# Attention and two MoE layers in one kernel: spaced-out weight pieces, a different top-2 pick, one float16 product for token numbers

## The chip, the cores and the metric

The kernel runs on one core of a Trainium2 chip. The metric is the device time of one execution in microseconds (us). The core has TensorE (PE), VectorE (DVE), ScalarE (ACT), GpSimd (POOL) and SyncE (SP), and 16 DMA engines. SP, ACT and POOL have each a queue from which they issue DMAs.

## The reference, cut to what matters

```python
# attention: block 32, window 16; 16 heads of 768 x 64
scores_l = scale * q @ k.T            # only |i - j| < 16
scores_s = scale * q @ k_sum.T + log(32)   # 24 block maxima of k
a = softmax([scores_l, scores_s]); x = a @ [v, v_sum]  # v_sum: block means of v
# MoE: 1536 tokens, 8 experts, top 2
logits = x @ w_gate
noise_scale = np.log1p(np.exp(x @ w_noise))
noisy_logits = logits + noise_scale * noise
top2 = np.argpartition(-noisy_logits, 2, axis=1)[:, :2]
# out[token] = sum over its two experts of weight * (relu(x @ w1[e]) @ w2[e])
# then a dense layer: h = x @ w_in; out = max(0.01 * h, h) @ w_out
```

## The kernel before

**Attention** goes over 8 pairs of heads (n = 0 to 7), each in three groups, so 24 steps c = 3n + g. In a step TensorE computes scores (`score`), turns the softmax output of the step before (`turn_probs`, L1231) and multiplies with the values of an earlier one (`weigh`, L1252); VectorE does maximum and normalisation, ACT exp. The values of a pair lie in `v_win`, one of three buffers. SP loads their windows (`load_windows`, L343); TensorE then takes block means of them inside a score step (`block_means`, L1200), VectorE copies these out, ACT issues three small DMAs that put them into rows (`mean_rows`, L689), and GpSimd copies the rows into `v_win` (L575). `weigh` of a pair's first group waits for that copy. For pair 7 the window is loaded at SP's step n = 5, the means belong to c = 19, and `weigh(21)` waits for GpSimd's copy. At the end come the turns of x for the gate, the last `turn_probs(23)`, `weigh(22)`, `weigh(23)` and the logits.

**SP's queue** is written out by hand. Beside its loads for pair n it issues the weight pieces of `PIECES_BESIDE[n]`; (e, c) is piece c of expert e, 512 KB, for experts 0 and 1 only. At even n it stores pair n - 1 of x, three stores of 256 KB each; pair 7 is stored last. A DMA gives its piece to whoever splits it into a high and a low part: GpSimd for expert 0 (`split_first`) and for pieces 3 and 7 of expert 1, and for the other six ACT (high part, L740), TensorE (difference by identity products, `second_low_part`, L1374 and L1375) and ACT again (low part out of PSUM, L746).

**Routing** follows the last logits (L961). VectorE computes softplus from exp and log of ACT, adds it to the logits, takes the eight largest of each token and tile (L991), then their indices (L994), and makes the one-hot `chosen` from them (L996). Running counts per expert (L1001) go to TensorE, which sums them over partitions: the counts (L1382) and the ranks (L1385, L1387; their bank also holds the third low part, so they wait for ACT's copy of it). TensorE runs the low parts 0 to 2 ahead of the counts and 3 and 4 behind the ranks. VectorE derives each token's slot (L1009 to L1025), tile and row of it, and compares with tile and row numbers: `one_tile`, two digits of the token number in `at_tile`, and `at_row` in four parts (L1034). 48 products of TensorE with them (24 copies by two digits, L1394) give `token_of`, the list of tokens per slot. Each part of `at_row` is waited for. Then TensorE does the last low part and 14 transposes of an identity (`keep_warm`).

**Tiles.** GpSimd gathers x by `token_of` (L605, L601); the tile loop over 31 tiles turns x (L1408), ACT casts the high part (L786), VectorE subtracts for the low part (L1064), and TensorE multiplies high by high, low by high and high by low (L1421). Tile 0 also waits for all six low parts of expert 1. After the tiles comes the dense layer. The instructions after the tile loop's start are the same in number before and after the change.

On VectorE `link` makes the next instruction wait for the one just issued; an instruction without it is followed at once.

## Time and profile before

| what | value |
|---|---|
| median of 3 runs | 790.65 us (790.47 to 792.28) |
| the profiled execution | 787.81 us |
| its span | 786.2 us |
| PE busy | 758.4 us (96%) |
| DVE, ACT, POOL busy | 264.1, 230.0, 368.7 us |
| HBM read, written | 75.43 MB, 23.59 MB |

Times inside the span are counted from its start. The profiled execution is one of its own, 2.84 us below the median of the runs. A busy TensorE is not TensorE at its peak, as its matmuls are pipelined. A releaser in square brackets is what ended the idle time before an instruction.

### The profile page before, as it was taken

How to read it: one execution, taken by the hardware profiler on the slowest of the kernel's cores; microseconds unless marked ns; L12 is line 12 of the kernel's file. 1: busy time of each engine (PE TensorE's matmuls, PEld its weight loads, DVE VectorE, ACT ScalarE, POOL GpSimd, SP SyncE). 2: the span in 40 equal slices, each digit the busy share in tenths (PEclk: the TensorE clock that was granted, in tenths of full speed). 3: DMA queues.
4: the chain of work that ended last, by engine and by line, in shares of the span. 5: the costliest groups of instructions: out<-in, count | busy, mean ns of one | idle time of the engine just before them, and what ended most of it. 6: DMA issues, size and time to landing. Idle time of an engine off the chain costs nothing.

```text
span 786.2 us, 13127 instructions
## 1 busy us (share of the span) xinstructions
PE 758.4 (96%) x4505; PEld 620.9 (79%) x4506; DVE 264.1 (34%) x481; ACT 230.0 (29%) x384; POOL 368.7 (47%) x313
## 2 busy tenths in 40 slices
PE   7887798999999999999999999999999999999998
PEld 6666656778888888888888888888888888888886
DVE  2787563212222122121221212245433334332223
ACT  3777562222221222212212122144222222222212
POOL 5488525568788787868388871920010001000000
PEclk8999899999999999999999999999999999999999
DMA  9989734994443725353353621462010101010001
GB/s 177 211 196 244 238 135 126 347 317 148 141 166 99 234 94 207 100 173 120 133 184 112 225 80 43 118 203 79 28 55 27 54 1 53 0 53 0 0 1 53
DMA packets 77041, 97.74 MB, mean 124 GB/s; under 512 B 45768, under 2 KB 49008, under 8 KB 76976
## 3 DMA queue, kind: packets, MB, share of 16 engines
q1 hardware_dynamic: 58832, 45.52, 20.9%
q0 software_dynamic: 12464, 43.79, 17.4%
q10 hardware_dynamic: 5712, 7.99, 2.7%
q8 instruction: 21, 0.34, 0.2%
q14 instruction: 12, 0.10, 0.0%
HBM read 75.43 MB, written 23.59 MB: 126 GB/s over the span
## 4 chain that ended last, share of the span: by engine, by line
PE 89%; DVE 4%; DMA 3%; ACT 2%; issue 1%; POOL 0%; ACTq 0%; SPq 0%; DVEq 0%; POOLq 0%
PE p L1421 43%; PE p L1507 6%; PE p L1509 6%; PE p L1508 6%; PE p L1522 5%; PE p L1524 5%; PE p L1523 5%; PE p L1413 3%; DMA v_win<-in_v 2%; PE p L1408 2%; PE p L1231 1%; ACT scores L659 1%; PE p L1252 1%; DMA mean_rows<-mean_parts 1%; DVE scores L869 1%
## 5 line engine op out<-in xcount | busy, mean ns | idle before, releaser
L558 POOL TENSOR_TENSOR w_lo<-stage,w_hi 128x1024 fp32r<-128x1024 f32 x56 | 134.2, 2396 | 4.7
L1421 PE MATMUL p<-w_hi,xT_hi 128*128 x248 | 99.3, 400 | 1.9 <-DVE xT_lo L1064 1.9
L1421 PE MATMUL p<-w_lo,xT_hi 128*128 x248 | 96.7, 390 | 0.0
L1421 PE MATMUL p<-w_hi,xT_lo 128*128 x248 | 96.7, 390 | 0.0
L1421 PE MATMUL p<-w_hi,hT_hi 128*128 x240 | 96.5, 402 | 0.0
L1421 PE MATMUL p<-w_lo,hT_hi 128*128 x240 | 93.9, 391 | 0.0
L1421 PE MATMUL p<-w_hi,hT_lo 128*128 x240 | 93.5, 390 | 0.0
L645 POOL DMA_INDIRECT y_pick<-y_by_tile,slots x20 | 19.2, 959 | 157.5 <-PE p L1494 132.4
L1507 PE MATMUL p<-f_xT_hi,w_hi 128*128 (+2 forms) x200 | 77.2, 386 | 0.8 <-DVE f_xT_lo L1108 0.8
L1509 PE MATMUL p<-f_xT_hi,w_lo 128*128 (+2 forms) x200 | 76.2, 381 | 0.0
L1508 PE MATMUL p<-f_xT_lo,w_hi 128*128 (+2 forms) x200 | 76.2, 381 | 0.0
L789 ACT CAST hT_hi<-p 128x1024 fp32r<-128x1024 f32 x30 | 30.5, 1015 | 154.9 <-PE p L1413 154.9
L1522 PE MATMUL p<-w_hi,f_hT_hi 128*128 128x512 f32 x192 | 74.8, 390 | 0.1
L1523 PE MATMUL p<-w_lo,f_hT_hi 128*128 128x512 f32 x192 | 74.7, 389 | 0.0
L1524 PE MATMUL p<-w_hi,f_hT_lo 128*128 128x512 f32 x192 | 74.7, 389 | 0.0
L1116 DVE SCALAR_TENSOR_TENSOR f_h<-p,f_h 128x512 f32<-128x512 f32 x48 | 33.2, 691 | 119.9 <-ACT f_h L819 119.9
L1064 DVE TENSOR_TENSOR xT_lo<-p,xT_hi 128x512 fp32r<-128x512 f32 x31 | 21.4, 691 | 149.7 <-ACT xT_hi L786 149.7
L784 ACT ACTIVATE h_row<-p 128x1024 f32<-128x1024 f32 x30 | 30.8, 1027 | 136.3 <-PE p L1421 136.3
L819 ACT COPY f_h<-p 128x512 f32<-128x512 f32 x48 | 28.2, 588 | 143.2 <-PE p L1509 143.2
L556 POOL TENSOR_SCALAR w_hi<-stage 128x1024 fp32r<-128x1024 f32 x56 | 59.1, 1056 | 16.1 <-DMA stage<-in_moe_w 13.4
L1070 DVE COPY y_row<-p 128x512 f32<-128x512 f32 x31 | 21.5, 694 | 115.9 <-PE p L1421 115.9
L1421 PEld LDWEIGHTS p<-w_hi,xT_hi 128*128 128x128 f32 x248 | 46.6, 188 | 11.0 <-issue 2.4
(227 smaller groups left out, 1283.4 us busy)
## 6 DMA issues: line engine op xcount, KB each, us to landing
stage<-in_moe_w POOLq DMA_DIRECT2D x48, 512.0 KB, 4.0
w_land<-in_moe_w SPq DMA_DIRECT2D x16, 512.0 KB, 6.8
y_by_tile<-y_row ACTq DMA_DIRECT2D x29, 256.0 KB, 2.0
x_by_tile<-x_ring SPq DMA_DIRECT2D x28, 256.0 KB, 5.0
x_row<-x_by_tile SPq DMA_DIRECT2D x28, 256.0 KB, 2.9
v_win<-in_v SPq DMA_DIRECT2D x8, 384.0 KB, 5.4
x_tokens<-x_out SPq DMA_DIRECT2D x12, 256.0 KB, 7.1
out<-f_y SPq DMA_DIRECT2D x9, 256.0 KB, 2.0
```

The costliest lines, as they stand in the source:

```text
L556: pool.tensor_scalar(w_hi[:, par, cols], stage[:, c % STAGES, :], 1.0, 1.0, ALU.mult, ALU.mult).then_inc(hi_split, 1)
L558: pool.tensor_tensor(w_lo[:, par, cols], stage[:, c % STAGES, :], w_hi[:, par, cols].bitcast(F32), ALU.subtract).then_inc(lo_split, 1)
L784: nc.scalar.activation(h_row[:], h_bank[:], ACT.Relu).then_inc(h_ready, 1)
L789: nc.scalar.copy(hT_hi[:].rearrange("p c m -> p (c m)"), hT_bank[:]).then_inc(hT_hi_ready, 1)
L1116: nc.vector.scalar_tensor_tensor(out=h, in0=f_h_bank[c % 2], scalar=0.01, in1=h, op0=ALU.mult, op1=ALU.max).then_inc(f_leaky_done, 1)
L1421: last = nc.tensor.matmul(bank, a, w, start=(c == 0 and i == 0), stop=(c == left_hi.shape[1] - 1 and i == 2))
L1507: nc.tensor.matmul(to, hi, f_xT_hi[:, cols], start=(k == 0), stop=False)
L1508: nc.tensor.matmul(to, hi, f_xT_lo[:, cols], start=False, stop=False)
L1509: last = nc.tensor.matmul(to, lo, f_xT_hi[:, cols], start=False, stop=(k == KD - 1))
L1522: nc.tensor.matmul(f_y_bank[m], f_hT_hi[:, c % 2, rows], hi, start=(c == 0), stop=False)
L1523: nc.tensor.matmul(f_y_bank[m], f_hT_hi[:, c % 2, rows], lo, start=False, stop=False)
L1524: last = nc.tensor.matmul(f_y_bank[m], f_hT_lo[:, c % 2, rows], hi, start=False, stop=(c == FC - 1))
```

## The change

It has five parts.

- SP issues pieces (1,3) and (1,4) only when the window of pair 7 has landed, (1,0) to (1,2) between the three stores of pair 5, and (1,5) to (1,7) when pair 7's mean rows have landed, ahead of the stores of pair 7.
- Softplus: instead of dividing by (1 + t) - 1 with a guard against zero, it subtracts ((1 + t) - 1 - t) / (1 + t) from the log. One addition moves ahead of the wait for exp.
- The picks: instead of indices, an equality with the largest and second largest value over 192 columns, a correction for ties, a running count (scan) over the same, and a product that keeps the first match.
- Slots and token numbers: first slots by a shifted view of the sums (one subtraction less, one memset more); the token number is one float16 value, so `at_tile` is one tensor op and there are 24 products; `keep_warm` after them has 8 transposes.
- The first tile's product takes all terms with x's high part first, and waits for the low part only then.

```diff
-        PIECES_BESIDE = [((0, 0), (0, 1)), ..., ((0, 7), (1, 3), (1, 4)), ((1, 0), (1, 1), (1, 2)), ((1, 5), (1, 6), (1, 7))]
+        PIECES_BESIDE = [((0, 0), (0, 1)), ..., ((0, 7),), (), ()]
+        PIECES_BEHIND_V = (3, 4)
+        PIECES_BETWEEN_STORES = (0, 1, 2)
+        PIECES_BEHIND_MEANS = (5, 6, 7)
...
+                if n == PAIRS - 3:
+                    sp.wait_ge(v_loaded[(PAIRS - 1) % VBUF], last_v)
+                    for c in PIECES_BEHIND_V:
+                        load_piece(1, c)
                 if n >= 1 and n % 2 == 0:
                     for g in range(GROUPS):
                         store_x(n - 1, g)
+                        if n == PAIRS - 2:
+                            load_piece(1, PIECES_BETWEEN_STORES[g])
+            sp.wait_ge(means_loaded[(PAIRS - 1) % VBUF], 16 * MEAN_LOADS * ((PAIRS + 1) // VBUF))
+            for c in PIECES_BEHIND_MEANS:
+                load_piece(1, c)
...
+            link(nc.vector.tensor_tensor(te(7), plain, te(0), ALU.add))
             dve.wait_ge(exp_done, 1)
             nc.vector.tensor_scalar_add(row(3), row(2), 1.0).then_inc(exp1_done, 1)
             dve.wait_ge(exp1_done, 1)
-            link(nc.vector.tensor_scalar_add(row(5), row(3), -1.0))
-            link(nc.vector.tensor_scalar(row(6), row(5), 0.0, None, ALU.is_equal))
-            link(nc.vector.tensor_tensor(row(5), row(5), row(6), ALU.add))
-            link(nc.vector.reciprocal(row(5), row(5)))
-            link(nc.vector.tensor_tensor(row(5), row(5), row(2), ALU.mult))
-            link(nc.vector.tensor_tensor(te(5), te(5), noise_sb[:], ALU.mult))
-            link(nc.vector.tensor_tensor(te(7), plain, te(0), ALU.add))
+            nc.vector.scalar_tensor_tensor(out=row(5), in0=row(3), scalar=-1.0, in1=row(2), op0=ALU.add, op1=ALU.subtract)
+            link(nc.vector.reciprocal(row(6), row(3)))
+            link(nc.vector.tensor_tensor(row(5), row(5), row(6), ALU.mult))
             dve.wait_ge(ln_done, 1)
-            link(nc.vector.tensor_tensor(row(6), row(6), row(4), ALU.add))
-            link(nc.vector.tensor_tensor(row(6), row(6), row(5), ALU.mult))
+            link(nc.vector.tensor_tensor(row(6), row(4), row(5), ALU.subtract))
+            link(nc.vector.tensor_tensor(te(6), te(6), noise_sb[:], ALU.mult))
             link(nc.vector.tensor_tensor(row(7), row(7), row(6), ALU.add))
...
-            for t in range(NT):
-                last = nc.vector.max_index(top8_at[:, t, :], top8[:, t, :], te(7)[:, t, :])
-            link(last)
-            link(nc.vector.tensor_tensor(chosen[:], iota_e..., top8_at..., ALU.is_equal))
+            nc.vector.tensor_tensor(tok(1), top8[:, :, 0], top8[:, :, 1], ALU.is_equal)
+            link(nc.vector.tensor_tensor(is_top[:], te(7)..., tops..., ALU.is_equal))
+            link(nc.vector.tensor_tensor(is_top[:, 1, :, 0], is_top[:, 1, :, 0], tok(1), ALU.subtract))
+            link(nc.vector.tensor_tensor_scan(flat_of(tops_so_far), same_pick..., flat_of(is_top), 0.0, ALU.mult, ALU.add))
+            link(nc.vector.scalar_tensor_tensor(out=flat_of(chosen), in0=flat_of(tops_so_far), scalar=1.0, in1=flat_of(is_top), op0=ALU.is_equal, op1=ALU.mult))
...
+            nc.vector.memset(tab_p[:, 2, 0:1], 0.0)
...
-            link(nc.vector.tensor_tensor_scan(g(2), ones[:, 0:E], g(1), 0.0, ALU.mult, ALU.add))
-            link(nc.vector.tensor_tensor(g(4), g(2), g(1), ALU.subtract))
+            link(nc.vector.tensor_tensor_scan(end_of, ones[:, 0:E], g(1), 0.0, ALU.mult, ALU.add))
...
-            nc.vector.tensor_tensor(at_tile[:, 0], one_tile[:], over(first_ids[:], TCOLS), ALU.mult)
-            nc.vector.tensor_scalar(at_tile[:, 1], one_tile[:], token_id[:, 0:1], None, ALU.mult)
+            nc.vector.tensor_tensor(at_tile[:], one_tile[:], over(token_ids[:], TCOLS), ALU.mult)
...
-                for digit in range(2):
-                    last = nc.tensor.matmul(token_bank, at_row[:, :, i], at_tile[:, digit, :, i], ...)
+                last = nc.tensor.matmul(token_bank, at_row[:, :, i], at_tile[:, :, i], start=(i == 0), stop=(i == 2 * NT - 1))
             last.then_inc(slots_done, 1)
             second_low_part(5)
-            keep_warm(14, p01[:, BANK:BANK + P])
+            keep_warm(8, p01[:, BANK:BANK + P])
...
+            def first_tile_product(w):
+                for half in range(2):
+                    for c in range(KD):
+                        hi, lo = w(c * F + 512 * half)
+                        for i, part in enumerate((hi, lo)):
+                            nc.tensor.matmul(h_bank[...], xT_hi[:, c, :], part, start=(c == 0 and i == 0), stop=False)
+                pe.wait_ge(xT_lo_ready, 1)
+                for half in range(2):
+                    for c in range(KD):
+                        last = nc.tensor.matmul(h_bank[...], xT_lo[:, c, :], w(c * F + 512 * half)[0], start=False, stop=(c == KD - 1))
+                return last
...
                 pe.wait_ge(w1_ready, loads)
-                pe.wait_ge(xT_lo_ready, t + 1)
-                first_product(w).then_inc(h_done, 1)
+                if age == 0:
+                    pe.wait_ge(xT_hi_ready, 1)
+                    first_tile_product(w).then_inc(h_done, 1)
+                else:
+                    pe.wait_ge(xT_lo_ready, t + 1)
+                    first_product(w).then_inc(h_done, 1)
```

The 16-bit tiles change from bfloat16 to float16. On GpSimd three small iotas at the start become one (`token_ids`), and the scan's mask `same_pick` is set by two memsets.

## Rows read from the trace of the kernel before

**Rows 1.** The page: busy us of TensorE (share of the span), instructions.

```profile
PE 758.4 (96%) x4505; PEld 620.9 (79%) x4506; DVE 264.1 (34%) x481; ACT 230.0 (29%) x384; POOL 368.7 (47%) x313
```

**Rows 2.** Timeline of SP's DMA issues, 50 to 130 us: start, us, what.

```profile
69.83 0.61 SPq L343 DMA_DIRECT2D v_win<-in_v  x1
...
85.56 1.61 SPq L350 DMA_DIRECT2D w_land<-in_moe_w  x3
```

**Rows 3.** Timeline, 64 to 106 us: start, us, engine, line, [idle before <-releaser].

```profile
79.34 1.20 PE L1200 MATMUL p<-v_win,half_sums 64*32 64x192 f32 x16 [2.87 <-DMA v_win<-in_v]
...
87.69 0.57 ACTq L689 DMA_DIRECT2D mean_rows<-mean_parts  x1
...
93.16 0.65 PE L1231 MATMUL p<-ident,scores 128*120 128x128 f32 x4 [0.22 <-ACT scores L659]
...
94.30 1.47 POOL L575 TENSOR_SCALAR v_win<-mean_rows 24x1536 f32<-24x1536 f32 x1 [7.34 <-DMA mean_rows<-mean_parts]
...
94.60 1.25 ACT L659 ACTIVATE scores<-scores,negmax 128x120 f32<-128x120 f32 x4 [0.17 <-DVE negmax L873]
...
95.83 0.69 PE L1252 MATMUL p<-v_win,probsT 120*64 120x65 f32 x16 [2.02 <-POOL v_win L575]
...
98.31 1.06 PE L1231 MATMUL p<-ident,scores 128*120 128x128 f32 x4
```

**Rows 4.** DMA queues of SP (q1) and ACT (q10): first 76:90, then 88:90.

```profile
q1 hardware_dynamic: 2314, 4.54, 97.8%
...
q10 hardware_dynamic: 1, 0.00, 0.1%
```

**Rows 5.** Windows: PE, PEld, DVE, ACT, POOL busy (count), then granted clock, DMA, GB/s.

```profile
98.00:99.00 1.00, 1.00 (x7) 0.97 (x5) 0.14 (x1) 0.44 (x1) 1.00 (x1) 0.50 0.00 0
...
125.00:126.00 1.00, 1.00 (x4) 0.48 (x2) 0.90 (x6) 0.00 (x0) 0.79 (x1) 0.50 0.00 0
```

**Rows 6.** Timeline of the routing, 106 to 128 us.

```profile
107.38 0.21 DVE L978 TENSOR_SCALAR r_sc<-r_sc 128x96 f32<-128x96 f32 x1
...
108.17 0.75 DVE L981 RECIPROCAL r_sc<-r_sc 128x96 f32<-128x96 f32 x1
...
110.71 0.92 DVE L991 MAX8 top<-r_sc 128x8 f32<-128x8 f32 x12
...
113.21 1.01 ACT L746 CAST w_lo<-p 128x1024 fp32r<-128x1024 f32 x1 [1.16 <-PE p L1375]
...
113.42 0.36 DVE L996 TENSOR_TENSOR chosen<-iota_e,top_at 128x192 f32<-128x192 f32 x1
...
114.17 0.36 DVE L1001 TENSOR_TENSOR_SCAN r_sc<-same_expert,r_sc 128x96 f32<-128x96 f32 x1
...
116.04 0.26 DVE L1016 TENSOR_TENSOR r_sc<-p,tab_p 128x96 f32<-128x96 f32 x1
...
119.05 0.41 DVE L1031 TENSOR_SCALAR at_tile<-one_tile,token_id 128x768 bf16<-128x768 bf16 x1
...
119.09 0.80 PE L1375 MATMUL p<-w_hi,minus_ident 128*128 128x512 f32 x1
119.37 2.17 DVE L1034 TENSOR_TENSOR at_row<-row_numbers,slot_b 128x768 bf16<-128x768 bf16 x4
...
119.98 3.53 PE L1394 MATMUL p<-at_tile,at_row 128*128 128x32 bf16 x48
...
124.62 1.16 POOL L605 DMA_INDIRECT x_first<-x_tokens,token_of  x1 [21.52 <-DVE token_of L1044]
...
127.28 1.01 ACT L746 CAST w_lo<-p 128x1024 fp32r<-128x1024 f32 x1 [4.81 <-PE p L1375]
```

**Rows 7.** The chain that ended last, around the first product.

```profile
128.96 0.45 PE p L1408 x4
...
130.05 0.70 DVE xT_lo L1064
...
131.00 5.76 PE p L1421 x24
```

More of the change, by code:

```diff
@@ L22 @@
 F32, F32R = mybir.dt.float32, mybir.dt.float32r
-I32, U32, BF16 = mybir.dt.int32, mybir.dt.uint32, mybir.dt.bfloat16
+I32, U32, F16 = mybir.dt.int32, mybir.dt.uint32, mybir.dt.float16
 ALU, ACT, AX = mybir.AluOpType, mybir.ActivationFunctionType, mybir.AxisListType
@@ L122, in build @@
         with ExitStack() as room:
[L123 to L125 removed]
+            row_numbers = sb("row_numbers", [P, P, 2 * NT], F16, where=room)
+            tile_numbers = sb("tile_numbers", [P, TCOLS, 2 * NT], F16, where=room)
+            token_ids = sb("token_ids", [P, 2 * NT], F16, where=room)
             before = sb("before", [P, P], where=room)
@@ L129, in build @@
             same_expert = sb("same_expert", [P, E, NT], where=room)
+            same_pick = sb("same_pick", [P, 2 * NT, E], where=room)
         stage = sb("stage", [P, STAGES, CW])
@@ L148, in build @@
         with ExitStack() as room:
-            sb("under_routing", [P, 2380], where=room)
+            sb("under_routing", [P, 2092], where=room)
             r_sc = sb("r_sc", [P, 12, NT * E], where=room)
@@ L501, in _ @@
             link(pool.memset(same_expert[:, :, 0], 0.0))
-            link(pool.iota(first_ids[:].rearrange("p (k t) -> p k t", k=2), [[0, 2], [P, NT]], base=0, channel_multiplier=0, allow_small_or_imprecise_dtypes=True))
+            link(pool.memset(same_pick[:], 1.0))
+            link(pool.memset(same_pick[:, :, 0], 0.0))
+            link(pool.iota(token_ids[:].rearrange("p (k t) -> p k t", k=2), [[0, 2], [P, NT]], base=0, channel_multiplier=1, allow_small_or_imprecise_dtypes=True))
             signal(pool.iota(tile_numbers[:], [[1, TCOLS], [0, 2 * NT]], base=0, channel_multiplier=0, allow_small_or_imprecise_dtypes=True))
@@ L992, in _ @@
             link(last)
-            for t in range(NT):
-                last = nc.vector.max_index(top8_at[:, t, :], top8[:, t, :], te(7)[:, t, :])
-            link(last)
-            link(nc.vector.tensor_tensor(chosen[:], iota_e[:].unsqueeze(1).unsqueeze(1).to_broadcast([P, 2, NT, E]),
-                                         top8_at[:, :, 0:2].rearrange("p t k -> p k t").unsqueeze(3).to_broadcast([P, 2, NT, E]), ALU.is_equal))
+            tops = top8[:, :, 0:2].rearrange("p t k -> p k t")
+            flat_of = lambda a: a[:].rearrange("p k t e -> p (k t e)")
+            nc.vector.tensor_tensor(tok(1), top8[:, :, 0], top8[:, :, 1], ALU.is_equal)
+            link(nc.vector.tensor_tensor(is_top[:], te(7).unsqueeze(1).to_broadcast([P, 2, NT, E]), tops.unsqueeze(3).to_broadcast([P, 2, NT, E]), ALU.is_equal))
+            link(nc.vector.tensor_tensor(is_top[:, 1, :, 0], is_top[:, 1, :, 0], tok(1), ALU.subtract))
+            link(nc.vector.tensor_tensor_scan(flat_of(tops_so_far), same_pick[:].rearrange("p a e -> p (a e)"), flat_of(is_top), 0.0, ALU.mult, ALU.add))
+            link(nc.vector.scalar_tensor_tensor(out=flat_of(chosen), in0=flat_of(tops_so_far), scalar=1.0, in1=flat_of(is_top), op0=ALU.is_equal, op1=ALU.mult))
             by_expert = lambda i: r_sc[:, i, :].rearrange("p (e t) -> p e t", e=E)
@@ L1034, in _ @@
                 nc.vector.tensor_tensor(at_row[:, :, copies], row_numbers[:, :, copies], over(slot_b[:, 1, copies], P), ALU.is_equal).then_inc(rows_known, 1)
-            link(nc.vector.tensor_scalar(g(5), g(2), 1.0 / P, None, ALU.mult))
+            link(nc.vector.tensor_scalar(g(5), end_of, 1.0 / P, None, ALU.mult))
             ft = lambda i: tab_f[:, i, 0:TILES]
@@ L1392, in _ @@
                     pe.wait_ge(rows_known, i // PART + 1)
-                for digit in range(2):
-                    last = nc.tensor.matmul(token_bank, at_row[:, :, i], at_tile[:, digit, :, i], start=(i == 0 and digit == 0), stop=(i == 2 * NT - 1 and digit == 1))
+                last = nc.tensor.matmul(token_bank, at_row[:, :, i], at_tile[:, :, i], start=(i == 0), stop=(i == 2 * NT - 1))
             last.then_inc(slots_done, 1)
             second_low_part(5)
-            keep_warm(14, p01[:, BANK:BANK + P])
+            keep_warm(8, p01[:, BANK:BANK + P])
             def turn_x(t, half=0, uses=0):
@@ L1427, in first_product @@
                     last = part_products(h_bank[:, 512 * half:512 * half + 512], range(KD), xT_hi, xT_lo, lambda c: w(c * F + 512 * half))
+                return last
[4 more added lines that the diff above has]
+                        for i, part in enumerate((hi, lo)):
+                            nc.tensor.matmul(h_bank[:, 512 * half:512 * half + 512], xT_hi[:, c, :], part, start=(c == 0 and i == 0), stop=False)
+                pe.wait_ge(xT_lo_ready, 1)
+                for half in range(2):
+                    for c in range(KD):
+                        last = nc.tensor.matmul(h_bank[:, 512 * half:512 * half + 512], xT_lo[:, c, :], w(c * F + 512 * half)[0], start=False, stop=(c == KD - 1))
                 return last
```

31 lines of the change are left out of this document (15 added, 16 removed).

## The prediction

> **What bounds the kernel now.** I began with the page: TensorE is busy for 96% of the span [rows 1]. A change pays only where TensorE waits, so I looked for its waits, and the list of waits and the chain of waits put nearly all of them ahead of the tile loop. From 131.00 us, where the first expert product starts [rows 7], TensorE hardly stops again, so what starts that product earlier moves the end by as much.
>
> Then the timeline of the end of attention. TensorE waits 2.87 us, until 79.34, for the last values' window, and 2.02 us, until 95.83, for GpSimd's copy of the last block means (L575), which itself waits for a DMA until 94.30 [rows 3]. That DMA was issued from ACT at 87.69, and in 88 to 90 one packet of its queue moved [rows 3, 4]. SP's queue was full: 4.54 MB in 76 to 90, 324 GB/s [rows 4]. The windows show the third cost: TensorE's granted clock is at 0.50, the 1.2 GHz level, in 98 to 99, after the second wait [rows 5].
>
> Last, the timeline of the routing, 106 to 131. It is a serial chain on VectorE, with TensorE beside it busy with the second expert's low parts; the two lists must be laid over each other, as the later one decides at each crossing.
>
> **Part 1, the paced pieces.** Ahead of the window load issued at 69.83 nothing changes in SP's order, and it is taken to be served in order: 9.5 us from issue to TensorE's start [rows 2, 3]. The first wait stays: 0. Behind it, three pieces (1,5) to (1,7), issued at 85.56 before [rows 2], come only after the means have landed. What is left behind the window: (0,7), mostly moved by 80.6, and then five pieces of 0.52 MB and three stores of 0.26 MB, 3.4 MB. By the 324 GB/s of [rows 4] that is 10.5 us from about 80.5: the queue is empty near 91 where it was empty near 94. The means then land near 91, GpSimd's copy of 1.47 us [rows 3] ends near 92.5, and TensorE reaches that product at 95.83 - 2.02 = 93.81. So the wait of 2.02 goes, with 1.3 us to spare. What is late next is the last softmax: TensorE's turn of it (L1231) waits for exps that ran from 94.60 for 1.25 [rows 3], so it starts at 95.9 and not 98.31: 2.4 us. Behind it the same work ran at the low clock (L1231 1.06 us, against 0.65 for the turn before [rows 3]); if the clock stays up, the transposes, this turn and the product after it give another 0.75. I take 3.15, because the low clock followed the wait; bounds 2.0 and 3.15.
> The moved pieces are covered: (1,5) is first read by ACT at 114, GpSimd reads (1,7) far later, and both would be in by 97. Pair 7's stores stand behind them on SP, but their data is ready only from 95.8. SP's new wait for the window holds up (1,3), (1,4) and the stores of pair 5, which nobody wants before 99. All 0.
>
> The Trainium skill, "DMA: Bandwidth & Descriptors", section "Queues, rings and completion order", says that an engine goes round-robin between its queue rows a packet at a time, so the SP backlog should hold the means up by a packet per turn and not by its whole length. The trace shows 6.6 us from the issue at 87.69 to the copy at 94.30 [rows 3]. By the rule alone part 1 would give less, which is the first rival.
>
> **Part 2, routing up to the counts.** Softplus: L978 to L980 took 107.38 to 108.17; now the moved add delays the start by 0.10 and one unlinked step of 0.18 follows, so the reciprocal (0.75) starts at 107.66, 0.51 earlier than 108.17 [rows 6]. From its start to L991's, 2.54 us, lay 0.79 for itself and six steps of 0.29; four are left: 0.58. L991 starts at 109.61, 1.10 earlier. Picks: from the end of L991 (111.63) to L996 (113.42) twelve index searches, 1.79, and L996, 0.36 with 0.04 of link, go. In come an is_equal over 12 values (0.10 unlinked), the is_equal over 192 (0.40, as L996), a fix on 12 (0.21), the scan over 192 and a product over 192 (0.40). The scan is not in the trace; over 96 it took 0.36 (L1001), a tensor op 0.26 (L1016), so per 96 values 0.10 more: 0.56 and a link 0.04 for 192. Bounds: 0.36 (no slower than L996) and 0.76. In all 1.71 for 2.19. The running counts, ready at 114.53, would be there 1.58 earlier, at 112.95.
> Here TensorE takes over. It is on the third low part until 113.17 (ACT's copy of it starts at 113.21 and lasts to 114.22 [rows 6]), so the count product starts at 113.2. The rank product wants that copy gone, as it writes the same bank: 114.3, and its two halves take 0.7, to 115.0. VectorE's table steps are over by 114.45, so the subtraction L1013 that goes and the memset that comes are hidden; if that cover were gone they would give 0.1 to 0.2. L1016 starts at 115.0 for 116.04: 1.04 gained, 0.75 of the 1.8 lost to TensorE and ACT.
>
> **Part 3, token numbers.** L1031 goes: 119.37 - 119.05 = 0.32. VectorE's row masks (L1034, 2.17 for four) then run 118.0 to 120.2. float16 is as wide as bfloat16, so I keep the durations; below that no reason for a gain, above it at worst L1034 twice as long, 2.2. TensorE's fourth and fifth low parts ended at 119.89 [rows 6]; they start with the ranks, 0.55 earlier, and end at 119.35. So the token product starts at 119.45, not at 118.6 when its first rows are known. It has 24 products and not 48: half of 3.53, 1.77. It ends at 121.2, when the last rows have been there for 1 us, and not at 123.51: 2.3 gained. GpSimd's first gather moves from 124.62 to 122.3; it was in before the turn of 128.96 [rows 7], so now by 126.6 at the latest.
> Then the sixth low part and the warming transposes, 8 for 14. Before, that part ended at 127.25 (ACT's copy starts at 127.28 [rows 6]), 3.74 us after the token product, at clock 0.50 in 125 to 126 [rows 5]. With the same 3.74 it ends at 124.95, ACT's copy at 126.0; fourteen transposes took 1.7, to 128.96 [rows 7], so eight take 1.0, to 125.95. The first tile's turn follows both, between 126.0 and 126.5. I take the later, as it waits for the copy's signal too: 2.5. Bounds: 2.9 if the clock stays up or the signal costs nothing, and 1.3 if it stays down through the transposes as well, each then twice as long.
>
> **Part 4, x's high part first.** The first product waited until 131.00 for xT_lo, which took 0.70 from 130.05, and 0.24 of signal [rows 7]. It now waits for xT_hi, which is there when xT_lo's work begins, and the same 0.24; the low products come after sixteen others, 3.8 us at 5.76 for 24, so xT_lo's 0.70 is covered by them: 0.7. The number of products is the same, and only for this tile.
>
> **Sum.** 3.15 + 2.5 + 0.7 = 6.35 us. The profiled execution took 787.81 us outside a span of 786.2; it becomes 781.5 (span 779.9). The runs' median is 790.65, 2.84 above; I take that distance as unchanged: 784.3. Nothing later gives it back as far as I see: the gathers for tile 3 on start with the token numbers too, 2.3 + 3.15 earlier.
>
> **The rivals.**
> 1. The means stay late, since the copy waits for the transfer's own turns among large packets and not for the backlog's end. For: the trace does not say which packets the means stood behind, and 3.4 MB are ahead of them still. Against: one packet in 88 to 90 [rows 4], and the landing at 94.30 just when the rest was through. Gain 3.2: 787.5.
> 2. The window load is not served in order, so the pieces behind it delayed it. Then the first wait of 2.87 and its low clock, some 1.5, go too: 779.9. Against: two pieces and three stores, 1.8 MB, stood ahead of it on SP (5.6 us at 324 GB/s), which with its own transfer fill the 9.5.
> 3. Routing gives little: the clock falls at another place, or ACT's copies decide. 0.9 for 3.2, total 4.0: 786.6.
> 4. Slower: with fewer warming transposes and a wait for the gather, the clock falls to 1.2 GHz as the first products begin. A tile's 24 products last 5.76 us [rows 7], 0.24 each; at half clock as much again. It turns the result when 27 products run low; over two tiles it is +11.5 - 6.35, or 795.8. Against: between the turn and the first product lay some 1.6 us without work before as well, and the products ran at 0.24, the high clock's pace.
> The Trainium skill, "TensorE: Matmul & The Clock Gate", says in its part on transposes that these do not count as busy for the clock gate in the same way. By it, 8 or 14 would matter little; the trace has the clock coming back during the 14, and no run here tells whether through them.
> 5. The change does nothing measurable, two parts falling short together: 789.5.
>
> **The numbers.** Forecast 0.62, rival 1 0.14, rival 2 0.06, rival 3 0.11, rival 4 0.03, rival 5 0.04. The forecast's own range by its bounds is 783.9 (3.15 + 2.9 + 0.7) to 786.7 (2.0 + 1.3 + 0.7). The range reaches past the lower for a partly shorter first wait and to rival 1: 782.4 to 787.6; it leaves out rivals 2, 4 and 5. No change is told from noise within 0.3%, 2.4 us: the forecast and rivals 1 to 3 are beyond it, rival 1 by 0.8 only, so part of it counts as same. Faster 0.89, same 0.08, slower 0.03.
>
> **What would show it.** In the changed profile: L1200's wait near 79.3 as before; no wait ahead of the third last L1252, with L575 starting near 91; a high clock in 94 to 98; L991 to the counts shorter by 0.5; the count product right behind a low part; 24 token products starting behind another low part; first product 6.3 us earlier, at 124.7. The prediction is wrong if the means still land at 94, or if a low clock stands over the first tiles.

## The result, and the profile after

The changed kernel takes 787.33 us, the median of 6 runs (785.75 to 787.85), against 790.64 us for the kernel before (790.32 to 792.28, 6 runs): the ratio over the runs is 0.9935, with a 95% interval of 0.9912 to 0.9959, or 3.2 to 7.0 us of 790.64. The medians alone are 3.3 us apart. The forecast was 784.3 with a range of 782.4 to 787.6, so the time lies at the range's upper end. The profiled execution took 787.29 us outside a span of 785.7; that of before took 787.81 and 786.2. These two profiles differ by 0.5 us, where the sum, made on the first, said 6.35. Where the rest went is the question of this part. The profile itself models the ends of TensorE's rows and does not measure them, which matters below.

The changed kernel's page, first part: busy us (share of the span), instructions. TensorE works 3.5 us less than in [rows 1].

```profile
PE 754.9 (96%) x4475; PEld 618.3 (79%) x4476; DVE 262.0 (33%) x457; ACT 230.0 (29%) x384; POOL 368.6 (47%) x313
```

The timeline of the changed kernel, SP's window load and the end of attention (start, us, engine, line; the lines are some 15 further down than before):

```profile
71.89 0.61 SPq L347 DMA_DIRECT2D v_win<-in_v  x1
...
80.98 0.86 PE L1215 MATMUL p<-v_win,half_sums 64*32 64x192 f32 x16 [2.09 <-DMA v_win<-in_v]
...
88.51 0.57 ACTq L704 DMA_DIRECT2D mean_rows<-mean_parts  x1
...
93.84 1.47 POOL L590 TENSOR_SCALAR v_win<-mean_rows 24x1536 f32<-24x1536 f32 x1 [4.59 <-DMA mean_rows<-mean_parts]
...
95.37 0.69 PE L1267 MATMUL p<-v_win,probsT 120*64 120x65 f32 x16 [0.73 <-POOL v_win L590]
...
97.16 0.60 PE L1246 MATMUL p<-ident,scores 128*120 128x128 f32 x4
...
104.07 0.26 DVE L976 TENSOR_TENSOR logits<-logits,p 128x96 f32<-128x96 f32 x1 [2.53 <-PE p L1312]
```

Against [rows 2, 3] the window load is issued 2.06 us later, before anything that the change touches. From there on things are sooner: TensorE's second wait is 0.73 us and not 2.02, and the turn L1246 takes 0.60 us and not 1.06. The last add to the logits starts 32.18 us after the window load's issue. In the kernel before that was 36.24 us (its row is below), so this stretch gave 4.06.

The windows of the same kernel (TensorE's busy us and count, granted clock, DMA share, GB/s). Nothing is at the low clock from 78 to 98 us, around the end of attention, but the first and the last row are:

```profile
12.00:20.00 8.00, 8.00 (x49) 0.50 1.17 193
...
78.00:98.00 20.00, 15.34 (x290) 1.00 0.74 248
...
132.00:134.00 2.00, 0.00 (x0) 1.00 0.90 306
134.00:142.00 8.00, 5.03 (x17) 0.57 0.99 328
```

The kernel before, the same kind of window near the start:

```profile
18.00:20.00 2.00, 2.00 (x30) 0.93 0.64 145
```

and, in its timeline, its last add to the logits and ScalarE's first write of h:

```profile
106.07 0.26 DVE L961 TENSOR_TENSOR logits<-logits,p 128x96 f32<-128x96 f32 x1 [2.53 <-PE p L1297]
...
136.78 1.02 ACT L784 ACTIVATE h_row<-p 128x1024 f32<-128x1024 f32 x1 [6.75 <-PE p L1421]
```

The row of 18 to 20 goes with the later start: before, TensorE was back at 2.4 GHz by then, in the changed kernel's execution it stood at 1.2 GHz until past 20. Apart from GpSimd's small tables at the start, the instructions up to there are the same in both. In the fourteen profiles of this study the window load's issue lies between 69.68 and 72.67 us with no order by kernel, and a second profile of the changed kernel has it at 70.05 us. These 2 us are chance.

The routing of the changed kernel, which answers to [rows 6]:

```profile
109.25 0.56 DVE L1010 TENSOR_TENSOR_SCAN tops_so_far<-same_pick,is_top 128x192 f32<-128x192 f32 x1
...
116.08 2.14 DVE L1049 TENSOR_TENSOR at_row<-row_numbers,slot_b 128x768 f16<-128x768 f16 x4
...
117.19 1.87 PE L1408 MATMUL p<-at_tile,at_row 128*128 128x32 f16 x24
...
120.17 1.16 POOL L620 DMA_INDIRECT x_first<-x_tokens,token_of  x1 [17.53 <-DVE token_of L1059]
```

The scan over 192 values, whose price the prediction had to guess, took the 0.56 us that it took for it. The 24 token products take 1.87 us. From the last logits to GpSimd's first gather it is 16.10 us, and was 18.55.

The chain that ended last, in the changed kernel, from the gather on:

```profile
120.17 3.49 DMA x_first<-x_tokens,token_of
...
125.30 3.93 PE p L1450 x16
129.23 1.82 PE p L1454 x8
...
131.49 5.48 issue
136.97 1.97 PE p L1427 x8
138.94 6.78 PE p L1435 x24
```

Here is the loss. In the kernel before the first product starts 24.93 us behind the last logits [rows 7], here 21.23, so 3.70 us more are won; all in all the first product starts at 125.30 and not at 131.00. But then 5.48 us pass with TensorE, by its rows, doing nothing, the eight transposes of h take 1.97 us, and the second tile's product starts at 138.94 and takes 6.78 us. Before, the transposes took 1.1 us, the second product started at 139.26 and took 5.75. Of 5.70 us ahead, 0.32 are left at its start.

The sum by stages, in us (both columns are profiled executions):

| stretch | before | after | gain | forecast |
|---|---|---|---|---|
| start to window load | 69.83 | 71.89 | -2.06 | 0 |
| window load to last logits | 36.24 | 32.18 | 4.06 | 3.15 |
| last logits to first product | 24.93 | 21.23 | 3.70 | 3.2 |
| first to second tile's product | 8.26 | 13.64 | -5.38 | 0 |

Behind it the second product costs 1.03 us more, and 1.36 come back at the entrance of the tile loop, where TensorE stood still in the kernel before (157.24 to 158.60) and does not here; that makes the 0.5 us of the spans within 0.2.

ScalarE waits for the same thing (the changed kernel's timeline, the rows of its engine):

```profile
124.46 0.59 ACT L801 CAST xT_hi<-p 128x512 fp32r<-128x512 f32 x1 [2.10 <-PE p L1422]
135.89 1.02 ACT L799 ACTIVATE h_row<-p 128x1024 f32<-128x1024 f32 x1 [10.85 <-remote]
```

The product's rows end at 131.05, and ScalarE, which waits for nothing but that end, starts at 135.89. "remote" says that the trace names nobody who ended the wait just then. Either the rows show a false end or ScalarE was held up by something else; the experiments had to say which.

### The profile page after: what moved, and what is told of

Its sections match the earlier page's. It is cut to its first block, busy times and chain, and to the rows that moved or that the text cites. A ratio compares the mean times of both kernels' runs of the same rounds, so it can differ in the third digit from the quotient of the medians.

```text
span 785.7 us, 13043 instructions
## 1 busy us (share of the span) xinstructions
PE 754.9 (96%) x4475; PEld 618.3 (79%) x4476; DVE 262.0 (33%) x457; ACT 230.0 (29%) x384; POOL 368.6 (47%) x313
## 4 chain that ended last, share of the span: by engine, by line
PE 90%; DMA 3%; DVE 2%; issue 2%; ACT 2%; POOL 0%; ACTq 0%; SPq 0%; POOLq 0%; DVEq 0%
PE p L1435 43%; PE p L1538 6%; PE p L1540 6%; PE p L1539 6%; PE p L1553 5%; PE p L1555 5%; PE p L1554 5%; PE p L1427 4%; DMA v_win<-in_v 2%; PE p L1422 2%; PE p L1389 1%; PE p L1246 1%; ACT scores L674 1%; PE p L1267 1%; DVE scores L884 1%
## 5 line engine op out<-in xcount | busy, mean ns | idle before, releaser
L1435 PE MATMUL p<-w_hi,xT_hi 128*128 x240 | 96.6, 402 | 0.0
L1435 PE MATMUL p<-w_hi,xT_lo 128*128 x240 | 94.0, 392 | 0.0
L1435 PE MATMUL p<-w_lo,xT_hi 128*128 x240 | 93.9, 391 | 0.0
L1435 PEld LDWEIGHTS p<-w_lo,hT_hi 128*128 128x128 f32 x240 | 45.0, 188 | 10.0
```

The costliest lines, as they stand in the source:

```text
L1435: last = nc.tensor.matmul(bank, a, w, start=(c == 0 and i == 0), stop=(c == left_hi.shape[1] - 1 and i == 2))
```

## The experiments

Times of one chip are compared with the kernel before on that chip, whose median there is given, since it is not the same on all of them. The letters of the theories belong to their set of experiments: B and C below are not the B and C of the later sets.

**The parts alone** (one chip, the kernel before at 792.0 us, 31 runs). The pacing alone is the hunk on the pieces; the routing alone is the hunks on VectorE and the token product; the high part first is the last two hunks:

```diff
-                pe.wait_ge(xT_lo_ready, t + 1)
-                first_product(w).then_inc(h_done, 1)
+                if age == 0:
+                    pe.wait_ge(xT_hi_ready, 1)
+                    first_tile_product(w).then_inc(h_done, 1)
```

> Only the paced pieces (part 1), the rest as before. In the changed kernel the stretch from the last window load on SP to the last logits took 32.2 us and not 36.2, so if that is all pacing's doing this kernel is 4.0 us faster: about 786.6. The first wait for the window stays at 2 to 3 us. Theory A (the 5.4 us lost between first and second expert product belong to the split first product): no loss here, gap between the two products as before, 2.5 us. Theory B (they belong to the gathers standing closer to the first product): none here either, as everything moves alike. Theory C (they hang on how long the instruction lists are ahead of them): no loss, TensorE's, VectorE's and ACT's lists are unchanged.

> Only routing and token numbers (parts 2 and 3, eight warming transposes), the rest as before. First product about 2.5 to 3 us after the logits sooner. Theory A: gap between first and second product stays 2.5 us, 787.8 in all. Theories B and C: the gap grows to about 8 us and the kernel is 2 to 3 us slower than before, 793.

> Only the first tile's product with x's high part first (part 4). Theory A: first product 0.7 us sooner, then a gap of about 8 us for 2.5, so about 5 us slower, 795. Theories B and C: 0.7 us sooner and nothing else, 790.0.

> The changed kernel without part 4: the first product waits for x's low part again. Theory A: the gap between first and second product is 2.5 us again, so 4.7 us faster than the changed kernel, 782.6. Theory B and C: the gap stays near 8 us, 788.0.

Measured: pacing alone 788.22 us, ratio 0.9969 (0.9938 to 1.0001); routing alone 788.71, 0.9952 (0.992 to 0.9985); high part first alone 793.06, 1.0027 (0.9999 to 1.0056); all but the high part first 784.13, 0.9915 (0.9879 to 0.995). ScalarE's first write of h, in the timelines of pacing alone, routing alone, high part first alone and all without it, in this order:

```profile
138.87 1.02 ACT L798 ACTIVATE h_row<-p 128x1024 f32<-128x1024 f32 x1 [11.39 <-remote]
```

```profile
135.60 1.02 ACT L785 ACTIVATE h_row<-p 128x1024 f32<-128x1024 f32 x1 [6.75 <-issue]
```

```profile
141.67 1.02 ACT L784 ACTIVATE h_row<-p 128x1024 f32<-128x1024 f32 x1 [10.89 <-remote]
```

```profile
134.60 1.02 ACT L799 ACTIVATE h_row<-p 128x1024 f32<-128x1024 f32 x1 [10.70 <-PE p L1435]
```

The late end is there with the pacing alone, whose product is in the old order, and in the kernel without the new order. So the split product does not cause it, and no single part does. Of the three theories none is left: all of them had the pacing alone end in time, and B and C had the routing alone end late. The times by themselves lean to A (793.06 us for its 795 and 784.13 for its 782.6), but their intervals are about 5 us wide.

In the kernel without the new order, part of the late end stands in the rows: its product runs at the low clock for its first 6 us. From the product's start to ScalarE's write of h (TensorE's busy us and count, clock, DMA share, GB/s):

```profile
124.88:134.60 9.72, 9.00 (x28) 0.69 0.88 256
```

What the late end does to the parts can be read off once each stretch is measured from its own beginning. From the last logits to ScalarE's write of h: 30.71 us before and 27.75 with the routing alone, where the product ends in time; 34.86 with pacing alone, 34.85 with the high part first alone, 31.71 with all but the high part first and 31.82 in the changed kernel, where it ends late. With a late end the routing is still worth 3.0 to 3.2 us, and the new order, in these profiles, nothing: its product starts 0.7 us sooner (24.21 us behind the logits for 24.93, 21.23 for 21.99) and ends at the same time.

**Marks inside the product** (with the next three on a second chip, the kernel before at 791.25 us, 35 runs). The 4th, 8th, 12th, 16th and 20th of the 24 matmuls each raise a semaphore that idle VectorE waits for:

```diff
+                        if c % 2:
+                            last.then_inc(probe, 1)
...
+            for i in range(5):
+                dve.wait_ge(probe, i + 1)
+                nc.vector.memset(logits[:, 0, i:i + 1], 0.0)
```

> The changed kernel with marks inside the first tile's first product: five of its 24 matmuls (the 4th, 8th, 12th, 16th and 20th) and its last each release a small write on VectorE, which is otherwise idle then. Nothing is left out of the computation. In the changed kernel's trace the product's records end 5.75 us after its start (125.30 to 131.05), ScalarE's next instruction starts only at 135.89 and nothing seems to run between. Theory S (slow product): the product really ran at half its recorded pace, so that the six marks come 1.75 us apart, the last some 10.4 us after the start; the gap is a product at 1.2 GHz whose records and whose clock row do not show it. Theory B (blocked afterwards): the marks come 0.9 us apart, at the pace of the records, and only the end is released 4.8 us late. Theory F (ScalarE is short of instructions): the six marks all come in time, the last 5.8 us after the start, and ScalarE alone starts late. Time: as the changed kernel, 785 to 789 us by all three.

Measured 789.41 us, 0.9966 (0.994 to 0.9991). The marks, in VectorE's timeline; the product starts at 124.74:

```profile
126.00 0.06 DVE L1099 MEMSET logits<- 128x1 f32 x1 [0.79 <-issue]
126.91 0.06 DVE L1099 MEMSET logits<- 128x1 f32 x1 [0.85 <-issue]
128.01 0.06 DVE L1099 MEMSET logits<- 128x1 f32 x1 [1.04 <-PE p L1456]
130.85 0.06 DVE L1099 MEMSET logits<- 128x1 f32 x1 [2.78 <-PE p L1462]
134.37 0.06 DVE L1099 MEMSET logits<- 128x1 f32 x1 [3.46 <-remote]
```

The sixth mark says nothing: it waited for the first count of the end's semaphore, and VectorE itself raises that once earlier. ScalarE, which waits for the second, starts at 135.09. So four matmuls took 0.91 us between the first and second mark, then 1.10, 2.84, 3.52, and the last four 0.72. All three theories fall. ScalarE is not the one that is late (F), the hold-up is in the middle and not at the end (B), and the product is not at half pace throughout (S): it begins at full pace and is then slower than half pace. The matmuls' own rows show none of it. The clock's row is 1.00 up to 132 us, where the fourth group is already slow, and it says 0.50 behind 134, where the last four matmuls take no longer than at the full pace:

```profile
128.00:132.00 4.00, 2.91 (x15) 1.00 0.81 244
132.00:134.00 2.00, 0.00 (x0) 0.88 0.90 309
134.00:138.00 4.00, 1.83 (x9) 0.50 0.91 325
```

**Cover for TensorE**, to test whether its idleness before the product is the cause:

```diff
-            keep_warm(8, p01[:, BANK:BANK + P])
+            keep_warm(18, p01[:, BANK:BANK + P])
...
                 if age == 0:
+                    keep_warm(6)
                     pe.wait_ge(xT_hi_ready, 1)
```

> The changed kernel with TensorE kept busy up to the first product: 18 idle transposes instead of 8 behind the last low part, until the gathered rows land, and 6 more while ScalarE makes the high part (0.13 us each, so 2.3 and 0.8 us, which fill the idle 1.61 and 0.87 us of the changed kernel's rows). Theory S with idleness as its cause: the product takes 5.8 us instead of 10.6, the second product no longer begins at the half clock, and the time falls by 5 us beside the changed kernel (782 us). Theory S with another cause (the clock falls in the low part already or at random), B and F: the same time as the changed kernel within 1 us, or up to 0.5 us more from a transpose that is still running when the rows land.

> The same cover without the order that begins with x's high part: 18 transposes before the rows land and 12 while both parts of x are made (1.6 us). Theory S with idleness as its cause: a first product of 5.8 us that starts 0.7 us later than in the kernel with the new order: 783 us, under the 784.1 us that the change without that order had (whose first product ran at half the clock for 6.8 us in its profile). If the order alone causes the late end: this one has none, and beats the covered kernel with the order by some 4 us. B and F: 784 us, as without the cover.

> The changed kernel once more, on the chip of the other three, to compare with and for a second profile. If the late end of the first product belongs to every execution: again ScalarE's write of h starts 10.5 to 11.5 us after its first high part of x ended, and the times lie together (785.75 to 787.85 us before). If it comes and goes with the clock's phase: half of the profiles without it, and single times as low as 781 us.

Measured: with the cover 788.92 us, 0.9967 (0.9944 to 0.999); the cover without the new order 789.37, 0.997 (0.9946 to 0.9994); the changed kernel again 787.6, 0.9959 (0.9932 to 0.9986). ScalarE's write of h in the two with the cover:

```profile
135.39 1.02 ACT L799 ACTIVATE h_row<-p 128x1024 f32<-128x1024 f32 x1 [12.19 <-remote]
```

```profile
139.97 1.02 ACT L799 ACTIVATE h_row<-p 128x1024 f32<-128x1024 f32 x1 [13.54 <-remote]
```

Idleness is not the cause: with no idle stretch over 0.6 us in front of it, the product ended even later behind the first gather's issue, 17.03 and 18.50 us, than the 15.6 to 15.7 us of the changed kernel's two profiles. The extra transposes bought nothing.

**Less cover, and two holds that held nothing** (the first chip again, the kernel before at 793.56 us, 24 runs). The holds were a wait for the first count of the product's semaphore ahead of GpSimd's gathers and of SyncE's stores; that count stands long before, so nothing was held (the fourth gather was issued at 122.65 as always). These two are the marked kernel twice more.

> The changed kernel with the marks of the run before (five inside the first product, one at its end), and GpSimd's gathers of the fourth and later tiles held back until that product has ended, so that only the first three gathers move data under it. With the gathers running, the marks came at 126.00, 126.91 and 128.01 us, at the pace of the records, and then at 130.85, 134.37 and 135.07: the product is held up from its ninth matmul or so. Theory G (the gathers' and their stores' traffic holds TensorE back): all six marks 0.9 us apart, ScalarE's write of h 7 us after its first high part began in place of 11.2. The whole time then falls by up to 4.8 us, or less where the fourth tile or the second expert's weights, which stand behind the gathers on GpSimd, come late. Theory N (TensorE is held up by the number of its own instructions, or by something that the gathers do not touch): the same pace of marks as before, ScalarE's write 11 us after its high part began.

> The same marks, the gathers as in the change, but SyncE's stores of the gathered tiles to DRAM (256 KB each, the first issued 2.1 us after the product's start) held back until the first product has ended. If it is the stores that hold TensorE back (the marks fall behind just after the first store was issued at 126.88 us): marks 0.9 us apart. If it is the gathers: the same late marks as without this hold. Time: the fourth tile's rows must be stored and loaded before the tile loop, so 787 to 790 us either way.

> The same marks, with none of the 8 idle transposes behind the last low part. 16 idle transposes more made the product end 1.4 us later measured from the first gather's issue (17.0 us against 15.6), 22 more without the new order 2.9 us later (18.5). Theory N (the number of TensorE's instructions behind the gathers sets the end): ScalarE's write of h some 14.9 us after the first gather's issue, 0.7 us sooner than with 8. Theory G: 15.6 us, as with 8, since the rows land no earlier. If idleness before the product slows it by the clock: the marks of the first matmuls already come at half the pace, 1.7 us apart.

Measured 788.74 us (0.9947, 0.9922 to 0.9971), 790.04 (0.996, 0.9939 to 0.9981) and 789.81 (0.9968, 0.9947 to 0.999). The marks of the first of them, after a start at 123.81:

```profile
125.74 0.06 DVE L1100 MEMSET logits<- 128x1 f32 x1 [1.45 <-issue]
127.44 0.06 DVE L1100 MEMSET logits<- 128x1 f32 x1 [1.65 <-PE p L1457]
128.49 0.06 DVE L1100 MEMSET logits<- 128x1 f32 x1 [0.98 <-issue]
129.45 0.06 DVE L1100 MEMSET logits<- 128x1 f32 x1 [0.91 <-PE p L1457]
132.99 0.06 DVE L1100 MEMSET logits<- 128x1 f32 x1 [3.48 <-remote]
```

and its windows over the product's first half (busy us of PE, PEld, DVE, ACT and POOL, then clock, DMA share, GB/s):

```profile
124.00:126.00 2.00, 2.00 (x6) 1.54 (x6) 0.34 (x2) 0.00 (x0) 1.70 (x2) 0.52 0.70 203
126.00:128.00 2.00, 2.00 (x7) 1.59 (x6) 0.06 (x1) 0.00 (x0) 1.39 (x3) 0.63 0.76 186
128.00:130.00 2.00, 2.00 (x10) 1.65 (x9) 0.12 (x2) 0.00 (x0) 1.56 (x2) 1.00 0.91 254
```

This is a ruler for the clock: where the row says 0.52 four matmuls take 1.70 us, where it says 1.00 they take 0.96, and then, with the row at 1.00 still, 3.54. Marks of the kernel with the stores' wait: 0.92, 0.91, 3.25, 3.56, and 1.43 to ScalarE's start. Without the 8 transposes: 0.92, 0.90, 1.72, 3.57, and 2.83. The slowest group takes the same 3.5 to 3.6 us in all four marked profiles, about a quarter of the full pace. Without the transposes the write of h came 16.41 us behind the first gather's issue, not 14.9, so the count of TensorE's own instructions does not set the end either.

**The gathers really held**, by a wait for the second count (a third chip, the kernel before at 785.95 us, 17 runs):

```diff
             pool.wait_ge(top_w_done, 1)
+            pool.wait_ge(h_done, 2)
             gather_tiles(FIRST, 2 * NT)
```

> The hold of the gathers again, now on the second count of the semaphore that the first product raises: VectorE raises it once on its own before, so that a wait for the first count held nothing back, in this run's two forerunners. The gathers of the fourth and later tiles (and so the stores behind them) now start only when the first product has ended; the marks stand as before. In the marked profiles so far, groups of four matmuls took 0.9 to 1.1 us at first (the full pace), and two of the later groups 2.8 to 3.6 us each, which is slower than the 1.71 us of the half clock, while the clock's row stands at 1.00; this lasted some 6 to 7 us and ended 14.8 to 16 us after the first gather was issued, whatever stood ahead of the product. Theory G (traffic of the gathers and stores): with only three gathers in flight under it the product runs through at 0.9 us a group and ends 5.8 us after its start, ScalarE's write of h starts 7 us after the first high part began. Theory C (TensorE slows down on its own, by what it did before): two groups of 3 us or more again, ScalarE's write some 11 us after its high part began, and a clock row of 0.50 from about then. Time: by theory G the product's end comes 4.8 us sooner but the fourth tile's rows start on their way (gather, store, load: 15 us in the changed kernel's trace) only behind it, so 785 to 790 us; by theory C 790 to 796 us, since they start 11 us later than in the change.

Measured 785.78 us, 0.9994 (0.9966 to 1.0022). The last mark, ScalarE's write of h and the first held gather:

```profile
131.95 0.06 DVE L1100 MEMSET logits<- 128x1 f32 x1 [0.85 <-PE p L1463]
...
132.83 1.02 ACT L801 ACTIVATE h_row<-p 128x1024 f32<-128x1024 f32 x1 [6.02 <-PE p L1463]
...
133.55 0.94 POOL L617 DMA_INDIRECT x_ring<-x_tokens,token_of  x1 [7.90 <-PE p L1463]
```

Every group takes 0.91 us, and the write comes 26.95 us behind the logits, 3.76 sooner than in the kernel before and 4.9 sooner than in the changed one. That is what theory G said. But this chip is another one, and it is some 6 us faster with the kernel before as well. A second place tells more. Near 495 us, late in the tile loop, GpSimd gathers again while TensorE works, and no kernel here touches that. The turn of h and ScalarE's copy behind it there, first in the changed kernel, then in the kernel before:

```profile
495.00 1.03 PE L1427 MATMUL p<-ident,h_row 128*128 128x128 f32 x8
...
498.70 1.01 ACT L804 CAST hT_hi<-p 128x1024 fp32r<-128x1024 f32 x1 [7.92 <-remote]
```

```profile
495.76 1.03 PE L1413 MATMUL p<-ident,h_row 128*128 128x128 f32 x8
...
496.83 1.01 ACT L789 CAST hT_hi<-p 128x1024 fp32r<-128x1024 f32 x1 [5.30 <-PE p L1413]
```

Before, the copy follows the transposes' rows at once; in the changed kernel 2.7 us behind them. The copy is 2.4 to 2.7 us late there in twelve of the fourteen profiles, among them the routing alone (493.73 and 497.26) and the high part first alone, whose instructions there are those of the kernel before. It is in time in two, that of the kernel before and that with the held gathers (495.81 and 496.88), which holds nothing at that place. So TensorE's hidden slowness at 495 is a matter of the execution or the chip, not of the change, and at 128 to 135 it may be the same. The hold and the chip were changed together, and which of them took the slow stretch away is not decided.

The gathers' traffic by itself does not slow the product; the traces show that without a further run. These are the 5.78 us from the product's start in the kernel before and in the routing alone, which both end in time, and in the changed kernel, which ends late (TensorE's busy us and count, clock, DMA share, GB/s):

```profile
131.00:136.78 5.78, 5.78 (x26) 1.00 0.82 230
```

```profile
129.83:135.60 5.77, 5.77 (x26) 1.00 0.80 223
```

```profile
125.30:131.08 5.78, 5.78 (x26) 1.00 0.81 229
```

The gathers are not held in any of the three, and the DMA engines are as busy. If the gathers have a part in the slow stretch, something else must come with them.

The hold may also cost something later: from the tile loop's first turn (155.88) to the end of the span it is 630.6 us with the gathers held, and 627.6 and 627.9 in the kernels before and after. TensorE stands still for 2.57 us ahead of that turn, and the clock's row is at 0.50 in 156 to 158. The median of the held kernel equals that of the kernel before on its chip, though in the profile its write of h comes 3.76 us sooner. The changed kernel without the hold was not run on that chip, so the price of the hold is not known.

## Why the prediction was right, and where it was not

The time is in the range, and it is faster, as said. That the number lies in the range is in part luck. It is 3.0 us off the forecast and 0.27 under the upper end, and that end had been set for means that stay late (rival 1), not for what took the time back, a loss behind the start of the first product. Two signs that the prediction had named as speaking against it are there in part: the copy of the means starts at 93.84 us, where the sign said 94, though counted from the window load's issue it comes 21.95 us behind for 24.47; and a low clock stands over the first tiles, 0.57 in 134 to 142. Step by step:

- **Part 1, the first wait** was to stay. It did: 9.09 us from the load's issue to TensorE's start, 9.51 before, and a wait of 2.09. The range of all fourteen profiles is 8.85 to 10.10.
- **Part 1, the means.** They were to be in near 91 and the wait to be gone. The copy started 5.3 us behind the last of ACT's three issues instead of 6.6, at 93.84, and a wait of 0.73 us stayed: half way to rival 1. The sum had 2.4 us for the wait and 0.75 for the clock. Like with like, between kernels whose row of 78 to 90 us is 0.86 and which have no second fall of the clock, the stretch from the load to the logits is 35.18 us unpaced (routing alone) and 32.88, 32.89 and 33.09 paced; between those whose row is 0.72 it is 35.83 unpaced (high part first alone) and 33.85 to 34.12 paced. That is 1.7 to 2.3 us. The rest of the 4.06 is mostly two falls of the clock that the kernel before's profile has and the changed one's has not, the second of them 1.06 us (36.24 for 35.18); the other two unpaced kernels wait for the means too and do not have the second fall. So the pacing was mis-sized as 3.15 and is about 2, at its lower bound; the 0.75 for the clock was not the change's to give.
- **Parts 2 and 3**, 2.5 us, were right, and with their steps: the counts' product starts in the shadow of ScalarE's copy, the token products are 24 in 1.87 us (1.77), L1049 takes 2.14 us, L1034 took 2.17. From the last logits to the first gather it is 18.52 to 18.56 us in the three kernels without them and 16.10 to 16.12 in ten of the eleven profiles with them (17.79 in the other). From the last logits to the first product it is 24.45 with the pacing alone, whose clock does not fall there, and 21.98 with the routing alone: 2.5. In the profiles of before and after it is 3.0 without part 4, since before the clock fell in 124 to 128. The gather's landing decided the turn, not the transposes as the sum had it, which made no difference.
- **Part 4**, 0.7 us, was right at the place where it was put, the start of the product (0.72 and 0.76 in two pairs), and wrong in the sum. It took the product's end to move with its start. With the slow stretch in it, the end comes at the same time in both orders. The run times hold no gain for it either: the high part first alone has the ratio 1.0027 (0.9999 to 1.0056), and under the cover the two orders are equal, so it is more likely a loss than a gain.
- **The step that failed** is "Nothing later gives it back as far as I see" together with "I take that distance as unchanged", of the 2.84 us between the profiled execution and the median. The sum was made on an execution whose first product ends in time (ScalarE waits 6.75 us for it); in the eleven profiles that end late the wait is 10.6 us or more. After the change the distance is 0.04 us, and 0.91 in the second profile. The routing alone, whose product ends in time too, has 2.82, which looks like a rule; but the kernel with the held gathers ends in time and its profiled execution lies 2.35 us above its median, and the late ones lie between 1.73 below (with the stores' wait) and 3.87 above (without the new order). The distance by itself does not tell whether a product ends late; it was only no constant to be carried over.
- **Rival 4** had the place right, the first products, and a pace of TensorE as the cause, but with a clock row of 0.50 and a price of 5.76 us a tile. Measured: 4.8 us in the first tile, and 0.9 and 1.0 in the transposes and the product behind it, where the row does say 0.50, with 1.36 us of it back at the tile loop's entrance. It had been given 0.03, against it the products of the kernel before's profile, which run at the high clock's pace.

Taken together, the parts are worth about 2 + 2.5 = 4.5 us with a late first product, and, if part 4's gain at the start survives in one that is not late, 0.7 more; no such pair was measured. The 3.2 to 7.0 us of the ratio's interval hold either sum. Whether the other executions of the kernel before have the slow stretch was not shown: none of them has a profile.

Is the kernel without part 4 the better one? Its ratio is the best of the study, 0.9915, but its interval (0.9879 to 0.995) overlaps the changed kernel's, 0.9935 (0.9912 to 0.9959) and 0.9959 (0.9932 to 0.9986). With the cover, the two orders are equal (0.9967 and 0.997). It is open.

What stays open besides: what slows TensorE. Excluded are its order of products, idleness before it, the number of its instructions, ScalarE, and the gathers' traffic as the only cause. Left are that traffic together with something else, and something of the chip or the execution. It would take the held and the unheld kernel on one chip that shows the stretch.

## What to carry to other kernels

Compare a profiled execution's time with the median of its kernel before a sum is built on it; if their distance is as large as a part of the sum, take a second profile, since the distance need not stay. Measure each stretch from its own beginning (load's issue to logits, logits to gather, gather to product) and over several profiles: the times at which the parts ended scattered by 3 us here, the stretch from logits to gather, but for one profile, by hundredths, though that from load to logits still by 2 us, with the clock. And where a wait ends with no releaser, put marks on an idle engine inside the work that it waits for.

## What the runs showed of the hardware

- TensorE can be slower than its lower clock while the clock's row says 1.00. Groups of four 512-column matmuls took 0.91 us at the row 1.00, 1.70 at 0.52, and 3.5 to 3.6 with the row at 1.00 again; the slow groups together lasted 5 to 8 us. The Trainium skill, "TensorE: Matmul & The Clock Gate", section "Seeing it yourself", warns that the gate's events in traces are unreliable on this chip and that it was seen stuck at a quarter. By the first of these the row of 1.00 is no proof, and the marks agree; the pace of the slow groups, 0.88 us a matmul for 0.227, would fit the second, for a much shorter time. No run here tells whether it was the gate.
- The rows of matmuls do not show it either. In the changed kernel they end at 131.05, and the end's waiter starts at 135.89. The true end is read off the engine that waits.
- The same kernel put the same load at 71.89 and 70.05 us in two executions, and over all fourteen profiles it lies at 69.68 to 72.67 us, with the clock's early stretch at 0.50 ending at different times.
- The same DMA load over the same product, 223 to 230 GB/s, went with a product in time in two profiles and a late one in a third.
- The kernel before had medians of 785.95, 791.25, 792.0 and 793.56 us in four sets of runs on three chips.
